# Expert stage of a fused attention, expert and mixing kernel: P is scaled by GpSimd, scores are issued three units ahead, projections and other matmuls stand between the units

## What is computed

```python
# 1: attention, 8 heads of 64, keys: the last 96 and the first 8, with a bias by distance
# 2: experts: top 2 of 4 by softmax gate w; every expert is a causal attention of its own
for e in range(4):
    q, k, v = x @ wq[e], x @ wk[e], x @ wv[e]
    a = softmax(causal(scale * (q @ k.T)))
    out += gate[e] * (a @ v @ wo[e])          # gate is 0 where e is not chosen
# 3: mixing over positions, then a ReLU network
h = xt @ U @ V                                # rank 32
u = x + h.T
return u + relu(u @ w_ch1) @ w_ch2
```

## Time and profile before

| what | value |
|---|---|
| runs | median 510.8 us (510.22 to 511.42, 3 runs) |
| profiled execution | 513.78 us, its span 512.0 us |
| busy, share of the span | TensorE matmul 89%, weight load 75%, VectorE 44%, ScalarE 35%, GpSimd 28% |
| chain that ended last | TensorE 68%, VectorE 11%, GpSimd 8%, ScalarE 6% |
| mean granted TensorE clock | 0.983 of full speed |

### The profile page before, as it was taken

One profiled execution on the slowest core, in us unless ns is written; L12 is line 12 of the kernel. 1 busy time (PEld: TensorE's weight loads), 2 busy tenths in 40 slices (PEclk: granted clock), 3 DMA queues, 4 the chain that ended last, 5 costly groups with the idle time before them and its releaser, 6 DMA issues.

```text
span 512.0 us, 8491 instructions
## 1 busy us (share of the span) xinstructions
PE 455.5 (89%) x3192; PEld 386.0 (75%) x3192; DVE 225.4 (44%) x664; ACT 180.0 (35%) x479; POOL 144.4 (28%) x206
## 2 busy tenths in 40 slices
PE   2887787899966988888899999999999999999997
PEld 1565565689945866666689988888888788888886
DVE  3567667844688475585525512222222212222212
ACT  0876666621354466556732301111111111111112
POOL 0688888710043000410052302222222112222210
PEclk9999999999997999969999999999999999999999
DMA  7976643011052020400030201111111112211103
GB/s 212 304 215 176 180 150 116 1 36 30 1 157 70 2 61 2 121 24 2 1 125 0 63 1 41 42 42 41 42 44 48 32 42 83 83 63 41 42 0 125
DMA packets 29418, 36.63 MB, mean 72 GB/s; under 512 B 9696, under 2 KB 17760, under 8 KB 29376
## 3 DMA queue, kind: packets, MB, share of 16 engines
q1 hardware_dynamic: 29376, 36.07, 24.2%
HBM read 29.77 MB, written 3.15 MB: 64 GB/s over the span
## 4 chain that ended last, share of the span: by engine, by line
PE 68%; DVE 11%; POOL 8%; ACT 6%; issue 4%; DMA 1%; SPq 1%; DVEq 0%; ACTq 0%
PE ps_s L1045 26%; PE ps_o L1045 16%; PE ps_t L1045 13%; POOL prob L469 5%; PE ps_o L1209 3%; DVE prob L723 3%; ACT prob L512 3%; PE ps_t L1193 3%; DVE prob L774 2%; PE ps_s L1177 2%; PE ps_o L1093 1%; DMA kpos<-in_kpos 1%; DVE seps L763 1%; PE ps_o L1285 1%; PE ps_t L1073 1%
## 5 line engine op out<-in xcount | busy, mean ns | idle before, releaser
L512 ACT ACTIVATE prob<-prob,smin 128x256 f32<-128x256 f32 (+3 forms) x144 | 77.7, 542 | 49.2 <-DVE smin L723 49.2
L436 POOL TENSOR_TENSOR fl<-fraw,fh 128x512 fp32r<-128x512 f32 x32 | 41.4, 1293 | 177.5 <-DVE fh L957 177.5
L678 ACT ACTIVATE hidh<-ps_o 128x768 fp32r<-128x768 f32 x32 | 26.0, 812 | 181.4 <-PE ps_o L1045 181.4
L1028 DVE SCALAR_TENSOR_TENSOR hidl<-ps_o,hidh 128x768 fp32r<-128x768 f32 x32 | 30.6, 957 | 95.3 <-ACT hidh L678 95.3
L469 POOL TENSOR_SCALAR prob<-prob,sinv,one 128x256 f32<-128x256 f32 (+1 forms) x96 | 50.9, 547 | 9.5 <-DVE sinv L748 9.5
L1045 PE MATMUL ps_s<-hidh,fl 128*128 128x512 f32 x128 | 50.5, 394 | 0.0
L1045 PE MATMUL ps_s<-hidl,fh 128*128 128x512 f32 x128 | 50.2, 392 | 0.0
L1045 PE MATMUL ps_s<-hidh,fh 128*128 128x512 f32 x128 | 50.1, 391 | 0.0
L957 DVE CAST fh<-fraw 128x512 fp32r<-128x512 f32 x32 | 13.6, 426 | 71.2 <-PE ps_t L1045 71.2
L1193 PE MATMUL ps_t<-ident,prob 128*128 128x128 f32 x168 | 27.0, 296 | 19.2 <-DVE prob L774 11.6
L1045 PE MATMUL ps_o<-xl,w01h 128*128 128x256 f32 (+1 forms) x128 | 43.3, 338 | 0.0
(11 more groups left out here) (172 smaller groups left out, 1050.9 us busy)
## 6 DMA issues: line engine op xcount, KB each, us to landing
fraw<-in_w SPq DMA_DIRECT2D x32, 256.0 KB, 2.6
wraw<-in_w SPq DMA_DIRECT2D x8, 512.0 KB, 3.6
kT<-in_k SPq DMA_DIRECT2D x16, 224.0 KB, 4.4
qT<-in_q SPq DMA_DIRECT2D x8, 384.0 KB, 3.7
vN<-in_v SPq DMA_DIRECT2D x8, 384.0 KB, 5.2
out<-prob SPq DMA_DIRECT2D x12, 256.0 KB, 2.8
vB<-in_v SPq DMA_DIRECT2D x8, 192.0 KB, 5.2
mkh<-mkh SPq DMA_DIRECT2D x8, 192.0 KB, 2.7
```

Source lines behind the costliest of these rows:

```text
L436: return pool.tensor_tensor(lo, raw, hi.bitcast(F32), ALU.subtract)
L512: act.activation(prob_s, prob_s, ACT.Exp, bias=smin[:, col:col + 1], scale=-1.0, accum_out=ssum[:, col:col + 1]).then_inc(done, 1)
L678: act.activation(hidh[:, f % 2, :], ps_o[:, 0:S], ACT.Relu).then_inc(hidh_done, 1)
L1028: dve.scalar_tensor_tensor(hidl[:, f % 2, :], ps_o[:, 0:S], 0.0, hidh[:, f % 2, :].bitcast(F32), ALU.max, ALU.subtract).then_inc(hidl_done, 1)
```

## The change

- **Normalising**: `m_scale` on GpSimd adds EPS, waits for a reciprocal by VectorE (`inverse_unit`), and multiplies P by inverse and gate in one instruction with two scalars. VectorE's five instructions per unit become one.
- **Scores**: q and k are held once, in float32 (`mq`, `mk`), for all 4 blocks. A score is one float32 matmul with 64 rows, the experts of a pair in the two halves. The high and low parts and the DMA copies across partitions go.
- **Order**: scores run three units ahead (`AHEAD`). The table `FILL` (unit, place, kind, argument) puts 26 pieces of matmul work between the units: "p" projections of blocks 1 to 3, each in three parts, "v" values of batch 1, "n" transposes of the output, "r" ranks and "m" mix of batch 0, "w" wo @ w_ch1 pieces 0 to 2. They all use one bank (`ps_fill`, the second of `ps_o`), so each waits until the one before it is copied out, mostly by VectorE (`fill_take`).
- **Evacuation**: transposes of both experts are packed in groups of four (`t_groups`), and the outputs are copied out every three units.
- **Splits of w_ch1**: GpSimd does them behind the scaling of units 4, 7, 10, 15, 17, 20, 21 and 22 (`W1_BEHIND`).

```diff
-PROJECT_AT = {NT * (pp - 1): pp for pp in range(1, B * EP)}
-GATES_AT = {1: 0, NT + 1: 1}
+FILL = [(-1, 1, "p", (1, "k")), (-1, 1, "p", (1, "q")), (0, 1, "p", (1, "rest")), (1, 0, "v", NT), (1, 1, "v", NT + 1),
+        (2, 1, "v", NT + 2), (3, 1, "v", NT + 3), (4, 1, "v", NT + 4), (5, 1, "v", NT + 5), (6, 0, "p", (2, "k")),
...
+        (17, 1, "m", 1), (18, 0, "m", 2), (18, 1, "w", 0), (19, 1, "w", 1), (20, 1, "w", 2), (22, 1, "n", 3)]
+W1_IN_FILL = 3
+GATES_1_AT = 8
+
+W1_BEHIND = {4: 0, 7: 1, 10: 2, 15: 3, 17: 4, 20: 5, 21: 6, 22: 7}
+AHEAD = 3
...
-        mqs = sb("mqs", [P, 2, 2, S], F32R, where=exp_)
-        mkh = sb("mkh", [P, 2, 2, S], F32R, where=exp_)
-        mkl = sb("mkl", [P, 2, 2, S], F32R, where=exp_)
+        mq = sb("mq", [P, B * EP, S], where=exp_)
+        mk = sb("mk", [P, B * EP, S], where=exp_)
...
+        ps_fill = ps_o[:, 512:1024]
...
-            for pp in range(B * EP):
-                for half, ready in ((mkh, qk_hi), (mkl, qk_lo)):
-                    for par in range(2):
-                        sp.wait_ge(ready, 4 * pp + par + 1)
-                        sp.dma_start(half[halves[1 - par], pp % 2, par, :].bitcast(F32),
-                                     half[halves[par], pp % 2, par, :].bitcast(F32)).then_inc(qk_dup, 16)
-                if pp == 1:
-                    for j in range(4):
-                        load_w1(j)
-                if pp == 3:
-                    load_w1(4)
-                    load_w1(5)
+            for j in range(W1P):
+                load_w1(j)
...
+            def m_scale(v):
+                b, pr, i = v // (EP * NT), v // NT % EP, v % NT
+                col = 2 * N_UNIT + 2 * v
+                pool.wait_ge(mexp_done, 2 * v + 2)
+                pool.tensor_scalar(seps[:, col:col + 2], ssum[:, col:col + 2], EPS, None, ALU.add).then_inc(msafe_done, 1)
+                pool.wait_ge(minv_done, v + 1)
+                pool.wait_ge(gate_step, GATE_STEPS * (b + 1))
+                for par in range(2):
+                    x = m_prob[(2 * v + par) % 6][:, 0:P * (i + 1)]
+                    e = 2 * pr + par
+                    pool.tensor_scalar(x, x, sinv[:, col + par:col + par + 1], gate[:, NT * b + i, e:e + 1], ALU.mult,
+                                       ALU.mult).then_inc(mnorm_done, 1)
+            def split_w1(j):
                 pool.wait_ge(w1_in[j % 2], 16 * (j // 2 + 1))
-                if j < 3:
-                    pool.wait_ge(qk_done, 4)
-                elif j < W1S:
-                    pool.wait_ge(qk_done, 8)
+                if j < W1S:
+                    pool.wait_ge(fill_done, fill_of("p", (1 if j < 3 else 3, "rest")) + 1)
                 else:
-                    pool.wait_ge(w01_done, j - W1S + 1)
+                    pool.wait_ge(fill_done, fill_of("w", j - W1S) + 1)
                 pool.tensor_copy(by_unit(w1h[j % W1S]), w1_raw(j)).then_inc(w1h_done, 1)
                 pool.wait_ge(w1h_done, j + 1)
                 lo_of(w1_raw(j), by_unit(w1h[j % W1S]), by_unit(w1l[j % W1S])).then_inc(w1l_done, 1)
+            for v in range(M_UNIT):
+                m_scale(v)
+                if v in W1_BEHIND:
+                    split_w1(W1_BEHIND[v])
+            pool.wait_ge(mnorm_done, 2 * M_UNIT)
...
-                for par in range(2):
-                    act.activation(mkh[halves[par], pp % 2, par, :], ps_k[halves[par], :],
-                                   ACT.Copy).then_inc(qk_hi, 1)
-                act.wait_ge(qk_done, 2 * pp + 2)
-                for par in range(2):
-                    act.activation(mqs[halves[par], pp % 2, par, :], ps_q[halves[par], :],
-                                   ACT.Copy).then_inc(qk_hi, 1)
...
+            take_queries()
+            for v in range(AHEAD):
+                m_exp(v)
+            gates_exp(0)
+            for v in range(M_UNIT + 2):
+                if v >= 2 and (v - 2) % 3 == 2:
+                    o_out(v - 2)
+                fill_hi(v - 1, 1)
+                if v < M_UNIT:
+                    mevac(v)
+                if v + AHEAD < M_UNIT:
+                    m_exp(v + AHEAD)
+                if v == GATES_1_AT:
+                    gates_exp(1)
+                fill_hi(v, 0)
...
-                k = (3 if gates is not None else 2) * u
-                dve.tensor_scalar(seps[:, two], ssum[:, two], EPS, None, ALU.add).then_inc(step, 1)
-                dve.wait_ge(step, k + 1)
-                dve.reciprocal(sinv[:, two], seps[:, two]).then_inc(step, 1)
-                dve.wait_ge(step, k + 2)
-                scale, at = sinv, col
-                if gates is not None:
-                    dve.tensor_tensor(wgt[:, 2 * u:2 * u + 2], sinv[:, two], gates, ALU.mult).then_inc(step, 1)
-                    dve.wait_ge(step, k + 3)
-                    scale, at = wgt, 2 * u
-                for par in range(2):
-                    x = slots[(2 * u + par) % len(slots)][:, 0:w]
-                    dve.tensor_scalar(x, x, scale[:, at + par:at + par + 1], None, ALU.mult).then_inc(done, 1)
+            def inverse_unit(v):
+                two = slice(2 * N_UNIT + 2 * v, 2 * N_UNIT + 2 * v + 2)
+                dve.wait_ge(msafe_done, v + 1)
+                dve.reciprocal(sinv[:, two], seps[:, two]).then_inc(minv_done, 1)
...
-            for v in range(M_UNIT + 2):
-                if v < M_UNIT:
-                    m_attend(v)
-                if v in GATES_AT:
-                    gates(GATES_AT[v])
-                if 1 <= v <= M_UNIT:
-                    m_normalise(v - 1)
-                if v - 2 in PROJECT_AT:
-                    project_lo(PROJECT_AT[v - 2])
+            def w01_lo(j):
...
+                    elif x[1] == "rest":
+                        dve.tensor_copy(mk[:, x[0], HI], ps_fill[:, 0:256]).then_inc(k_out, 1)
+                        dve.tensor_copy(mq[:, x[0], HI], ps_fill[:, 256:512]).then_inc(q_out, 1)
+                    elif x[1] == "k":
+                        dve.tensor_copy(mk[:, x[0], LO], ps_fill).then_inc(k_out, 1)
+                    else:
+                        dve.tensor_copy(mq[:, x[0], LO], ps_fill).then_inc(q_out, 1)
...
+            for v in range(AHEAD):
+                m_attend(v)
+            gates(0)
+            inverse_unit(0)
+            fill_take(-1, 1)
+            inverse_unit(1)
+            for v in range(M_UNIT + 1):
+                if v:
+                    fill_take(v - 1, 1)
+                if v + 2 < M_UNIT:
+                    inverse_unit(v + 2)
+                if v + AHEAD < M_UNIT:
+                    m_attend(v + AHEAD)
+                if v == GATES_1_AT:
+                    gates(1)
+                fill_take(v, 0)
...
-                    w = (i + 1) * P
-                    slot = (b * EP + pr) % 2
-                    for k, cols in enumerate(PIECES):
-                        z = min(w, cols.stop)
-                        if z > cols.start:
-                            for keys, first in ((mkh, True), (mkl, False)):
-                                last = pe.matmul(ps_s[:, score_banks(r)[0] + k, 0:z - cols.start],
-                                                 mqs[:, slot, par, i * P:(i + 1) * P],
-                                                 keys[:, slot, par, cols.start:z], start=first, stop=not first)
...
+                w = (i + 1) * P
+                pieces = [(k, cols.start, min(w, cols.stop)) for k, cols in enumerate(PIECES) if w > cols.start]
+                for k, a, z in pieces:
+                    for par in range(2):
+                        half = slice(64 * par, 64 * par + 64)
+                        last = pe.matmul(ps_s[:, score_banks(2 * v + par)[0] + k, 0:z - a],
+                                         mq[half, pp, i * P:(i + 1) * P], mk[half, pp, a:z], start=True, stop=True)
+                        if k == pieces[-1][0]:
+                            last.then_inc(ms_done, 1)
...
+            for n in range(NT):
+                if n == 2:
+                    m_scores(0)
+                    m_scores(1)
+                project_values(n)
+            pe.wait_ge(xl_done, X_PARTS * HP * B)
+            m_scores(2)
+            fill(-1, 1)
             for v in range(M_UNIT + 1):
-                if v + 2 < M_UNIT:
-                    m_scores(v + 2)
-                if v and v % NT == 0:
+                if v < M_UNIT:
+                    m_transposes(v, slice(0, 2))
+                if v + AHEAD < M_UNIT:
+                    m_scores(v + AHEAD)
+                if v < M_UNIT:
+                    m_transposes(v, slice(2, None))
+                fill(v, 0)
+                if v:
                     m_values(v - 1)
-                if v in PROJECT_AT:
-                    project(PROJECT_AT[v])
-                if v < M_UNIT:
-                    m_transposes(v)
-                if v % NT:
-                    m_values(v - 1)
+                fill(v, 1)
...
+            last_weights(3)
+            fill_emptied(len(FILL) - 1)
```

(9 more changed lines are left out.)

558 lines of the change are left out of this document (287 added, 271 removed), and 2 rows, old and new, of the table FILL.

## The result

| | before | after |
|---|---|---|
| median of the runs | 511.11 us (510.22 to 511.49, 4 runs) | 498.44 us (496.69 to 499.22, 4 runs) |
| profiled execution, span | 513.78 us, 512.0 us | 499.12 us, 497.3 us |
| busy, share of the span | TensorE 89%, VectorE 44%, ScalarE 35%, GpSimd 28% | TensorE 91%, VectorE 38%, ScalarE 33%, GpSimd 37% |

The ratio is 0.9741, 95% interval 0.9714 to 0.9767: the change is faster by 12.7 us; 13.8 were forecast. A second measurement of the same kernel (`r0_after_again`) gave 497.83 us (496.45 to 499.22), ratio 0.9736 (0.9706 to 0.9765). Executions of one kernel differ in their clock: of the eight of the changed kernel four have a mean granted clock of 0.983 (498.7 to 499.2 us) and four 0.997 (496.5 to 497.8 us), and the profiles of both kernels are of an execution at 0.983, before's 2.7 us above its median and the changed kernel's 0.7.

A forecast was written before the change was run, and what follows sets the result against it. TensorE's 22.6 us of standing still in the expert stage, plus lower clock after waits, was what could be won. 31.3 regained less 11.5 new waits and 6.0 shape changes gave 13.8 us faster: median 497.0 us, range 486 to 508.

The forecast's parts named there:

- shape changes: TensorE, expert stage: 35 more switches between scores, transposes and values, at 0.17 us each, cost 6.0 us.
- hidden ends: TensorE, expert stage: groups ending in a wait are drawn too long; 22 waits hide 0.15 us each, 3.3 us.
- Comes back: Expert stage: 31.3 us regained, from old TensorE waits 22.5, lower clock 5.5 and drawn wait ends 3.3.
- new waits: Expert stage: the new fixed order makes TensorE wait 11.5 us, at the start, units 8-11, 13-14, 21-24 and elsewhere.
- The upper end: TensorE's shape changes: each costs 0.17 + 0.24 us, 14.4 us in all, leading to 505.4 us.
- Scores at nothing: TensorE's scores: float32 matmuls on half the rows, side by side, take 18.9 against 19.5 us, counted as zero.
- the rival's price: Rival on TensorE's scores, chance 0.07: the halves do not run side by side, costing 17.4 us, giving 514.4.
- GpSimd's load: GpSimd in the expert stage: 768 columns of scaling take 1,014 ns; 68 us busy of some 168, not the bound.
- Units 8 to 11: Batch 1's gates on VectorE, beside a GpSimd split, delay unit 11's P: 3.0 us of waits, one collision adding 2.4.
- Nothing for ScalarE: Expert stage: no new TensorE waits counted for ScalarE's copies; their return was named as how the size could be wrong.
- The waits stay covered: Rival, chance 0.17: copies and splits find TensorE busy, only 3.0 us of waits at the end remain, giving 488.5.
- GpSimd and VectorE take turns: Rival, chance 0.14: VectorE's work queues behind GpSimd's eight splits, costing 18.6 us instead of 6.0, giving 509.6 or more.

The follow-up runs named there:

- e5: The changed kernel with all transposes of a unit together before the scores of the unit three ahead: 501.74 us, ratio 0.9796.
- e8: The kernel before, its order and scores kept, with EPS and scaling of P on GpSimd and five splits between the scalings: 511.82 us, ratio 0.9976.
- e7: The changed kernel with all scores on rows 0 to 63, the second expert's own scores left out: 509.77 us, ratio 0.9981.
- e1: The changed kernel with the third split of w_ch1 behind unit 11 instead of unit 10: 500.1 us, ratio 0.9778.
- e9: The changed kernel with the gates of batch 1 behind unit 10's mask instead of unit 11's on VectorE: 496.38 us, ratio 0.9694.
- e11: e10 with sum + EPS formed on VectorE, right before the reciprocal, instead of on GpSimd: 493.34 us, ratio 0.9641.
- e6: The changed kernel with each split of w_ch1 cut to one row of 2 columns, loads and waits kept: 492.3 us, ratio 0.9622.
- e10: e9 plus three moves in VectorE's order (masks of units 0 and 1, block 1's k copy, second output-transpose copy): 493.86 us, ratio 0.9648.

## Why the prediction was right, and where it was not

The median of 498.4 us lies 1.4 from the forecast and well inside the range. By the forecast's terms, with differences of the unrounded values:

| term | forecast | measured, from the account |
|---|---|---|
| TensorE standing still | -22.5 + 11.5 = -11.0 | 22.6 to 10.4: -12.3 |
| clock | -5.5 | 6.7 to 4.2: -2.5 |
| work: shape changes + 6.0, hidden ends - 3.3 | + 2.7 | 154.4 to 155.5: + 1.1 |
| sum of the stage | -13.8 | -13.6 |
| rest of the span | 0 | 328.3 to 327.2: -1.1 |

**The step that failed is the clock.** "Comes back" took all 5.5 us, though the same text had new waits of 11.5 us in it. Behind two of the new waits the clock is at its lower level again: for 7.0 us from the 3.12 us wait of unit 10 on, and for 3.6 us from the 1.76 us wait of the output transposes on. 3.0 us of gain were counted that did not come. The work came out 1.6 us and the standing still 1.3 us better than forecast, which made up for it by luck: the sum is better than its parts. No trace was taken of an execution at a clock of 0.997, so how much of the 4.2 us such an execution loses is not shown.

**A second luck is in the step to the median.** Between the profiled executions the forecast was 13.8 us (500.0) and 14.7 came (499.1), 1.1 of it outside the stage. Between the medians 12.7 came. The forecast took the median 3.0 us below the profiled execution, as before; it lies 0.7 below. So 0.9 too little and 2.3 too much leave the 1.4 us.

- **Shape changes, 6.0, too high.** The work grew by 1.1 us. The waits fell from 22 to 11, which by the prediction's own 0.15 takes 1.7 off; so the new changes, with the scores at nothing, cost 2.8 us. Their number was near: TensorE's records show 54 before and 91 after, 37 more where 35 were counted (two too many for the third groups, as e5 shows, and some at the other pieces too few). That is 0.08 each. The account is good to a us or two between different programs (e8, with the matmuls of before, has 1.8 more than before), so the ends are 0.02 and 0.13; e5, where almost nothing else differs, gives 0.08. The 0.17 us gap of the weight load is there, but it does not cost its full length; that the matmuls before it are still running in it is the likely reason, and was not tested. The upper end (0.41 each), and with it what the prediction made of the rule of the Trainium skill (TensorEngine Tiling (Array Packing), Key Properties), does not hold here: if switching drains TensorE, the drain shows at about 0.1 us or less.
- **Scores at nothing: right.** e7 shows that it rests on the halves' running side by side, and the rival's price of 17.4 us was right (17.7).
- **GpSimd's load: right.** 987 ns for 768 columns against 1,014, and 68.2 us busy in the stage against 68. TensorE waited 0.2 us for it; the "waits for GpSimd's P at units 11 and 23, 1 to 3 us each" did not come.
- **The new waits.** Start: 1.7 + 1.1 = 2.8 against 2.2, but 1.1 of it is another wait (unit 2's scores behind VectorE's copies of value tiles and two masks), which wasn't counted. Units 8 to 11: 3.1 against 3.0, and the collision costs the gate step 2.1 where 2.4 was foreseen (2.32 instead of 0.25 us), but it reaches TensorE through ScalarE, whose order has the exponential of the gates ahead of the copy. Units 13 and 14: 1.8 for the transposed outputs as told, and 0.5 for the bank behind a copy of q, 2.3 against 2.6. Units 21 to 24: 1.04 + 0.21 + 0.23 + 0.15 = 1.6 against 3.0; the last splits are covered better than counted. Elsewhere 0.4 against 0.7.
- **"Nothing for ScalarE"** was wrong, as the text feared: 4.6 of the 10.2 us are for its copies, not because it is busy, but because it waits for VectorE with the copy behind it. The chains of e1, e9 and e11 all end in it.
- **The rivals.** "The waits stay covered" (488.5) did not come: it left 3.0 us of waits, and 10.2 stayed. Even e6 and e10, 492 and 494 us, still have some 8 us of standing still. "GpSimd and VectorE take turns" is a right mechanism at the wrong price: e6 puts all that the splits cost at 6.1 us, where the forecast had counted 6.0 and the rival 18.6. Its text named the gate steps as the only blocked kind of the new kernel's instructions, and the trace agrees; e11 adds that the sum, had it stayed on VectorE, would be of that kind too, as L763 was the earlier trace rows.

## What to carry to other kernels

Moving an operation to a slower, idle engine and giving the work more lead are one change, not two: here each alone was worth nothing and both together 12.7 us. When a wait is priced, price its clock with it, old and new alike. Look along every engine's fixed order for what stands behind the held instruction: in e1 and e9 TensorE was late for a copy whose input had long been there, queued behind an exponential that waited for a mask that waited for a reciprocal. Book the stage as standing still, clock and work; these three numbers told in every run which of them an edit had moved.

## What the runs showed of the hardware

- **A small VectorE instruction can wait out a whole one of GpSimd's.** A tensor_tensor of 96 columns took 2.32 instead of 0.25 us, a tensor_scalar of 2 columns 2.22 instead of 0.16, a pair of scalings of 640 columns 3.61, each beside GpSimd's subtraction of 1,024 columns (2.4 to 2.5 us). The reciprocal kept its 0.17 us beside a cast, a mask of 384 columns its 0.55 beside the subtraction, and a copy of 512 columns out of ps_o its 0.69. The Trainium skill says this of the port that both share (SBUF — State Buffer, Who interferes with whom), and the traces agree.
- **Two halves of TensorE's rows work independently.** The same scores took 1.35 or 1.36 us whether the halves alternated or each issued its two pieces in turn, and 2.43 us on one half.
- **The clock can fall behind a single wait, and the same wait need not do it.** In the changed kernel the lower level starts with the 3.12 us wait and with the 1.76 us wait at 213.7 us. e9 has the same 1.76 us wait, and the clock stays at 1.00 there; the 1.74 us wait for block 1's k has it in no kernel. A wait of 2.34 us stands before 0.93 (165 to 190 us) in e9 and before 1.00 in e10, one of 2.23 us before 0.93 in e11. In e6, with nothing over 1.74 us and 8.0 in all, it was 1.00 in the whole stage. And executions of one and the same kernel have a mean of 0.983 or 0.997. So neither the length of a wait nor the kernel alone decides it; what does stays open.
